# A slot's first four transposes moved ahead of the preceding slot's second product, and eight gate rows loaded sooner

## The chip, the cores and the metric

One core of one Trainium2 chip runs the whole kernel. The metric is the device time of one launch in microseconds (us). The kernel before the change has a median of 386.7 us over 3 runs (385.82 to 386.99).

The core's engines run side by side, each working through its own list of instructions in order and waiting on semaphores: TensorE (PE, matrix products and transposes into the eight banks of PSUM), VectorE (DVE), ScalarE (ACT), GpSimd (POOL) and SyncE (SP, which here only issues DMA transfers).

## The reference, cut to what matters

Three stages in a row on a batch of 2 x 768 tokens with 384 features:

```python
# 1: linear attention with a decaying 48x48 state per head (8 heads); x is [2, 768, 384] after it
state = w * state + k_t v_t;  y_t = r_t (state + u k_t v_t)
# 2: layer norm, then a hidden layer of 1536, added to x
x = x + relu(((x - mu) / sqrt(var + 1e-6) * g_ln) @ w_ch1) @ w_ch2
# 3: a mixture of 8 experts with a hidden layer of 1024
logits = x @ w_gate;  local = sigmoid(x @ w_local)
e[s] = argmax(logits[s]) if s == 0 or local[s] < 0.5 else e[s-1]
out[s] = softmax(logits[s])[e[s]] * (relu(x[s] @ w1[e[s]]) @ w2[e[s]])
```

## The kernel before, in words

Tokens are worked in 12 tiles of 128. Weights and activations are split into a high part (rounded to fp32r) and a low part (the difference, in the code `hi` and `lo`), and each product is three: high by high, low by high, high by low.

**First stage and hidden layer.** Two tiles are a group; there are six groups (0 to 5). On TensorE a group (`group`) makes eight blocks of the first product (`hidden`, L1033, pairs q = 0 to 7), with the attention products of later tiles between them, and then the second product for each of its two tiles (`rows_out`, L933 to L935). Each block q of the first product goes to one of two PSUM banks in turn. ScalarE makes its high part (L731), VectorE its low part (L1560), and only then may TensorE write block q + 2 into that bank. So block 2 of a group waits for VectorE's low part of block 0. GpSimd works meanwhile on the attention inputs of later tiles (`decays`, `rows`, `ends`).

**Gates.** The nine gate products of a token tile (eight experts and the local gate) are made on VectorE in `gates` (L1668): one `scalar_tensor_tensor` of 128 x 384 with an accumulated sum for each gate row, from the finished tile `x2` and the gate rows `wgr` broadcast to all partitions. VectorE's list is written out by hand, and gates are put in where it is thought to have time. For tile 0 the first five are at the start of group 1, ahead of `hidden(1, 0)`; for every later even tile the first four are in `rows_done`, between `turned` and `residual(g, 1)`.

**The gate rows** are loaded by SyncE in one transfer of nine rows (L469) into the first part of `stage`. That buffer held the pieces of `w_ch1` and `w_ch2` before; so the load waits for the semaphores `lo_v` and `lo_p`, by which VectorE and GpSimd tell that the low parts of all pieces are made. On SyncE's queue it stands behind the loads of tiles 4 and 5 and ahead of the stores of `x2`.

**Experts.** Tokens are gathered into slots of 128 that belong to one expert. Two early slots run beside the routing; then up to 18 slots (numbered from 0) run in a list that is cut off when no slot is live any more: with these inputs slots 0 to 13 are. From slot 9 on each slot's parts for the next one stand in an `If` on a value read from a table. In slot s TensorE does, in this order:

- `turn_rows(s+2)`: three transposes of gathered rows into bank 0 (L1318)
- `hidden_e(s+1, 0)`: nine products for the first half of the next slot's inner rows, into bank 2 (L1331, L1335, L1338)
- `turn_hidden(s)`: eight transposes of this slot's inner rows `he`, four into bank 4 and four into bank 5 (L1348)
- `hidden_e(s+1, 1)`: nine products for the other half of the next slot's inner rows, into bank 3
- `rows_out_e(s)`: the slot's second product, 24 matmuls into bank 6 (L1359, L1363, L1367)

Before four transposes are written into bank 4 or 5, `turn_hidden` waits for `he_ready` (ScalarE has made that half of `he`, L880) and for `heT_ready`, which counts VectorE's low parts (L1945): these read the same bank.

ScalarE in slot s (`slot`, L892 and after): the rows of slot s + 2 out of bank 0 (`turned_rows`, L872), the high parts of the two halves of the transposed rows (L902), two pieces of the next expert's weights rounded if its expert is new (`prepare`, L811), both halves of `he` for slot s + 1 (`hidden_rows`, L880), and two more pieces (L811).

VectorE in slot s: the low part of the rows of slot s + 2 (`turned_rows`, L1915), the low parts of the two halves of the transposed rows (L1945), two low parts of pieces if they are due (`prepare`, L1923), the output rows scaled (L1954, which waits for the end of `rows_out_e(s)`), and two more low parts of pieces if they are due (L1923). In slot 0 the code of the routing (`main_parts`) and `rest_e(1, EP)` (L1630) stand ahead of this list.

Of the kernel before, what the change touches and what calls it, by code (L numbers as in the profile page):

```python
# [15 lines left out]
P = 128  # L16
B, H, S, D = 2, 8, 768, 48
DM = H * D
# [9 lines left out]
F1 = 4 * DM  # L28
# [3 lines left out]
NG = NT // G  # L32
E = 8
# [19 lines left out]
LO_V = 2, 3, 5  # L53
LO_P = 5
GATED = (NG - 2) * G + 1
NSPENT = 6
# [56 lines left out]
def build_program(nc, consts, w_heads, u_row, r_t, k_t, r_rows, k_rows, v_rows, g_cols, w_ch1, w_ch2,  # L113
# [4 lines left out]
    with ExitStack() as ctx:  # L118
# [3 lines left out]
        def sem(name):  # L122
            return ctx.enter_context(nc.semaphore(name))
# [11 lines left out]
        ident = const("ident")  # L135
# [13 lines left out]
        at = WB + NT * DM  # L149
# [113 lines left out]
        p_got_e, p_slot_e = late([3, NEARLY]), late([NEARLY])  # L263
        xe = [xg[i].rearrange("p (k t) -> p k t", k=KD) for i in range(NEARLY)]
        heT_e = late([KF2, P])
        wgr = stage[:, 0:(E + 1) * DM]
        spent = [stage[:, (E + 1 + i) * DM:(E + 2 + i) * DM] for i in range(NSPENT)]

        parts_e = parts[:].rearrange("p (b w c) -> p b w c", b=2, w=2)

# [9 lines left out]
        s_zero, s_scan, s_wk, s_wr, s_we, s_uw, s_ng, s_eps = sems("s_zero s_scan s_wk s_wr s_we s_uw s_ng s_eps")  # L280
        rkT_ready, coef_mm = sems("rkT_ready coef_mm")
        s_pair, s_k1, s_hi0, s_wc = sem("s_pair"), sem("s_k1"), sem("s_hi0"), sem("s_wc")
        s_mean0, s_k2, s_gr, s_spent = sem("s_mean0"), sem("s_k2"), sem("s_gr"), sem("s_spent")
        s_v = [sem(f"s_v{u}") for u in range(2)]
        s_piece = [sem(f"s_piece{i}") for i in range(NPIECE)]
        s_warm = sem("s_warm")
# [95 lines left out]
        def when(eng, live, step):  # L382
            if live is None:
                step()
            elif live is not False:
                with eng.If(live > 0):
                    step()
# [11 lines left out]
        def _(sp):  # L399
# [17 lines left out]
            def load(c, u):  # L417
                load_turned(c, u)
                load_rows(c, u)
# [42 lines left out]
                sp.wait_ge(x2_ready, t + 1)  # L462
                sp.dma_start(x2_dram[bass.ds(t * P, P), :], x2[u]).then_inc(x2_out[u], 16)

            for u in range(2):
                load(4 + u, u)
            sp.wait_ge(lo_v, len(LO_V))
            sp.wait_ge(lo_p, LO_P)
            sp.dma_start(wgr, gate_rows.to_broadcast([P, (E + 1) * DM])).then_inc(s_gr, 16)  # L469
            for u in range(2):  # L470
                store(u, u)
            with sp.Fori(1, NG - 2) as g:
# [204 lines left out]
        def _(act):  # L677
# [194 lines left out]
                act.activation(xnT_hi[:, :, s % 2 * P:(s % 2 + 1) * P],  # L872
                               bk[0][:, 0:DM].rearrange("p (k t) -> p k t", k=KD), ACT.Copy).then_inc(xgT_hi_ready, 1)

            def hidden_rows(s):
                for half in range(2):
                    act.wait_ge(he_mm, 2 * s + half + 1)
                    if half == 0:
                        act.wait_ge(*((heT_mm, 2 * s) if s else (heeT_mm, 2 * NEARLY)))
                    act.activation(he[:, half * 512:(half + 1) * 512], bk[2 + half][:], ACT.Relu).then_inc(he_ready, 1)  # L880
# [12 lines left out]
            def slot(s, live):  # L893
                if s + 2 < NSLOT:
                    when(act, live, lambda: turned_rows(s + 2))
                if s + 1 < NSLOT:
                    read_name(s + 1)
                for half in range(2):
                    act.wait_ge(heT_mm, 2 * s + half + 1)
                    if half == 0:  # L900
                        act.wait_ge(*((ye_mm, s) if s else (yee_mm, NEARLY)))
                    act.activation(heT_hi[:, 4 * half:4 * half + 4, :].rearrange("p a t -> p (a t)"), bk[4 + half][:],  # L902
                                   ACT.Copy).then_inc(heT_hi_ready, 1)
                if s + 1 < NSLOT:
                    prepare(name[s + 1], range(EP))
                when(act, live, lambda: hidden_rows(s + 1))
                if s == 0:
                    round_e(1, EP + 1)
                else:
                    prepare(name[s], range(EP, 2 * EP))  # L910
# [10 lines left out]
        def _(pe):  # L921
# [399 lines left out]
            def hidden_e(s, e, half):  # L1321
                b = e if isinstance(e, int) else e & 1
                if half == 0:
                    pe.wait_ge(xgT_hi_ready, s + 1)
                pe.wait_ge(e_hi[0], e * EP + (half + 1))
                if s >= 1:
                    pe.wait_ge(he_ready, 2 * s + half - 1)
                u = slice(s % 2 * P, (s % 2 + 1) * P)
                hi, lo = (lambda k, w=w: e_cols(b, w, half * F1 + k * 512, 512) for w in range(2))
                for k in range(KD):  # L1330
                    pe.matmul(bk[2 + half][:], xnT_hi[:, k, u], hi(k), start=k == 0, stop=False)  # L1331
                if half == 0:
                    pe.wait_ge(xgT_ready, s + 1)
                for k in range(KD):
                    pe.matmul(bk[2 + half][:], xnT_lo[:, k, u], hi(k), start=False, stop=False)  # L1335
                pe.wait_ge(e_lo[0], e * EP + (half + 1))
                for k in range(KD):
                    mm = pe.matmul(bk[2 + half][:], xnT_hi[:, k, u], lo(k), start=False, stop=k == KD - 1)  # L1338
                mm.then_inc(he_mm, 1)

            def turn_hidden(s):
                for half in range(2):
                    pe.wait_ge(he_ready, 2 * s + half + 1)
                    if s >= 1:
                        pe.wait_ge(heT_ready, 2 * s + half - 1)
                    for f in range(4):
                        at = (4 * half + f) * P
                        mm = pe.transpose(bk[4 + half][:, f * P:(f + 1) * P], he[:, at:at + P], ident)  # L1348
                    mm.then_inc(heT_mm, 1)

            def rows_out_e(s, e):
                b = e if isinstance(e, int) else e & 1
# [26 lines left out]
            def slot(s, live):  # L1379
                if s + 1 < NSLOT:  # L1380
                    expert[s + 1] = pe.value_load(slot_tab[0:1, 0, s + 1:s + 2], min_val=0, max_val=E - 1)

                def ahead():
                    if s + 2 < NSLOT:
                        turn_rows(s + 2)
                    hidden_e(s + 1, expert[s + 1], 0)

                when(pe, live, ahead)
                turn_hidden(s)
                when(pe, live, lambda: hidden_e(s + 1, expert[s + 1], 1))  # L1390
                if s == 0:
                    lanes_main()
                rows_out_e(s, expert[s])
# [4 lines left out]
            hidden_e(0, 0, 0)  # L1398
            turn_rows(1)
            hidden_e(0, 0, 1)  # L1400
            pe.wait_ge(rt_v, RT_TABLES)
            live_slots(pe, slot)


        @block.vector
        def _(dve):
# [253 lines left out]
            def gates(t, columns):  # L1660
                dve.wait_ge(x2_ready, t + 1)
                if t == 0:
                    dve.wait_ge(s_gr, 16)
                for e in columns:
                    n = t * (E + 1) + e
                    if n >= NSPENT:
                        dve.wait_ge(s_spent, n - NSPENT + 1)
                    dve.scalar_tensor_tensor(spent[n % NSPENT], x2[t % 2], 1.0, wgr[:, e * DM:(e + 1) * DM],  # L1668
                                             ALU.mult, ALU.mult, accum_out=lg[:, t, e:e + 1]).then_inc(s_spent, 1)

            def group(g, ends=True):
                t0, t1 = (g - 1) * 2, (g - 1) * 2 + 1
                gates(t0, range(0 if g == 1 else 4, 5))
                hidden(g, range(0, 1))
                if not ends:
                    coefs(g * 2 + 2, 0)
                masked(g * 2 + 2, bk[0:2], scT[0])
                gates(t0, range(5, 7))
                hidden(g, range(1, 2))
                if ends:  # L1680
                    coefs(g * 2 + 2, 0)
                gates(t0, range(7, 8))
                hidden(g, range(2, 3))
                if ends:
                    new_state(g * 2 + 2, 0, bk[3])
                rows_of(g * 2 + 2, 0, bk[4])
                if not ends:
                    coefs(g * 2 + 3, 1)
                masked(g * 2 + 3, bk[0:2], scT[0])
                if ends:  # L1690
                    coefs(g * 2 + 3, 1)
                gates(t0, range(8, E + 1))
                hidden(g, range(3, 4))
                gates(t1, range(0, 1))
                hidden(g, range(4, 5))
                if ends:
                    new_state(g * 2 + 3, 1, bk[3])
                rows_of(g * 2 + 3, 1, bk[4])
                means(g + 1)
                gates(t1, range(1, 2))  # L1700
                hidden(g, range(5, NHP))
                gates(t1, range(2, E + 1))
                rows_done(g)

            def rows_done(g):
                if isinstance(g, int) and g == NG - 2:
                    dve.wait_ge(s_rest, 16)
                    flags(0)
                residual(g, 0)
                turned(g + 1)  # L1710
                if 0 < g < NG - 2:
                    gates(g * 2, range(0, 4))
                elif g == NG - 2:
                    gates(g * 2, range(0, 6))
                residual(g, 1)
                scales(g + 1)
                if g == NG - 2:
                    gates(g * 2, range(6, E + 1))
# [333 lines left out]
```

## Time and profile before

| what | value |
|---|---|
| median of 3 runs | 386.7 us |
| the profiled execution's own time | 387.67 us |
| its span in the profile | 385.8 us |
| TensorE busy | 372.7 us, 97% of the span |
| VectorE busy | 281.7 us, 73% |
| ScalarE busy | 155.4 us, 40% |
| GpSimd busy | 136.2 us, 35% |
| share of the chain that ended last | TensorE 89%, VectorE 6% |
| granted TensorE clock | full in nearly every slice |

The span is what the profile shows from the first to the last instruction. Every engine has a busy time; what matters is which engine the others wait for, and in which stretch. Here TensorE is busy nearly all the time, so the places where it sits idle are few.

### The profile page before, as it was taken

How to read it: one execution, taken by the hardware profiler on the slowest of the kernel's cores; microseconds unless marked ns; L12 is line 12 of the kernel's file. 1: busy time of each engine (PE TensorE's matmuls, PEld its weight loads, DVE VectorE, ACT ScalarE, POOL GpSimd, SP SyncE). 2: the span in 40 equal slices, each digit the busy share in tenths (PEclk: the TensorE clock that was granted, in tenths of full speed). 3: DMA queues.
4: the chain of work that ended last, by engine and by line, in shares of the span. 5: the costliest groups of instructions: out<-in, count | busy, mean ns of one | idle time of the engine just before them, and what ended most of it. 6: DMA issues, size and time to landing. Idle time of an engine off the chain costs nothing.

```text
span 385.8 us, 8869 instructions
## 1 busy us (share of the span) xinstructions
PE 372.7 (97%) x3056; PEld 338.9 (88%) x3056; DVE 281.7 (73%) x630; ACT 155.4 (40%) x281; POOL 136.2 (35%) x114
## 2 busy tenths in 40 slices
PE   8999989999999999999999999999999999999992
PEld 6889989999999999999999656789999999999981
DVE  7899769897898788769868568698646853647440
ACT  6556312212231321241441254368525852555520
POOL 2999772931760470100004006303332233223231
PEclk9999999999999999999999999999999999999997
DMA  7995633300511331400028495798875297101111
GB/s 216 337 338 167 198 129 111 113 20 25 169 44 42 109 109 41 165 3 22 20 83 292 136 309 141 262 369 308 297 274 160 76 286 286 39 22 48 20 47 42
DMA packets 32778, 56.67 MB, mean 147 GB/s; under 512 B 3277, under 2 KB 20339, under 8 KB 32608
## 3 DMA queue, kind: packets, MB, share of 16 engines
q1 hardware_dynamic: 30432, 49.84, 39.5%
q0 software_dynamic: 2304, 6.30, 5.6%
q8 instruction: 23, 0.38, 0.4%
q14 instruction: 19, 0.16, 0.1%
HBM read 51.41 MB, written 5.51 MB: 148 GB/s over the span
## 4 chain that ended last, share of the span: by engine, by line
PE 89%; DVE 6%; issue 2%; DMA 1%; ACT 1%; POOL 0%; SPq 0%; DVEq 0%; POOLq 0%; ACTq 0%
PE bank L1033 17%; PE bank L933 7%; PE bank L935 7%; PE bank L934 6%; PE bank L1359 5%; PE bank L1331 5%; PE bank L1367 5%; PE bank L1363 5%; PE bank L1338 5%; PE bank L1335 5%; PE bank L1348 3%; PE bank L1260 3%; PE bank L1237 3%; PE bank L948 3%; PE bank L979 2%
## 5 line engine op out<-in xcount | busy, mean ns | idle before, releaser
L1033 PE MATMUL bank<-xnT_hi,parts 128*128 128x256 f32 x432 | 65.5, 288 | 1.7 <-DVE parts L1560 1.4
L1033 PEld LDWEIGHTS bank<-xnT_hi,parts 128*128 128x128 f32 x432 | 56.6, 191 | 4.0 <-DVE parts L1560 1.9
L731 ACT ACTIVATE parts<-bank 128x512 fp32r<-128x512 f32 x36 | 21.5, 597 | 91.9 <-PE bank L1033 91.8
L1668 DVE SCALAR_TENSOR_TENSOR stage<-stage 128x384 f32<-128x384 f32 x81 | 56.4, 738 | 0.2
L665 POOL DMA_INDIRECT out_y<-late x14 | 20.5, 1461 | 93.9 <-DVE late L1954 93.9
L933 PE MATMUL bank<-parts 128*128 128x384 f32 x144 | 49.2, 342 | 0.0
L935 PE MATMUL bank<-parts 128*128 128x384 f32 x144 | 48.3, 335 | 0.0
L934 PE MATMUL bank<-parts 128*128 128x384 f32 x144 | 48.2, 334 | 0.0
L811 ACT ACTIVATE parts<-stage (+1 forms) x32 | 46.2, 1485 | 0.2 <-DMA stage<-in_w 0.2
L1923 DVE TENSOR_TENSOR parts<-stage,parts x24 | 41.1, 1755 | 4.9 <-ACT parts L811 4.2
L1033 PE MATMUL bank<-xnT_lo,parts 128*128 128x256 f32 x216 | 37.3, 282 | 0.0
L1560 DVE SCALAR_TENSOR_TENSOR parts<-bank,parts 128x512 fp32r<-128x512 f32 x36 | 24.8, 690 | 17.0 <-ACT parts L731 16.6
L572 POOL TENSOR_TENSOR arena<-arena,coef 128x384 f32<-128x384 f32 x12 | 13.0, 1080 | 62.3 <-DVE coef L1450 62.0
L1954 DVE TENSOR_SCALAR late<-bank,late 128x384 f32<-128x384 f32 x14 | 8.6, 618 | 32.6 <-PE bank L1367 32.5
L658 POOL DMA_INDIRECT late<-x_rows,late x18 | 22.3, 1240 | 28.2 <-DVE late L1880 23.0
L1033 PEld LDWEIGHTS bank<-xnT_lo,parts 128*128 128x128 f32 x216 | 30.9, 191 | 0.0
L933 PEld LDWEIGHTS bank<-parts 128*128 128x128 f32 x144 | 27.1, 188 | 0.1
L934 PEld LDWEIGHTS bank<-parts 128*128 128x128 f32 x144 | 27.1, 188 | 0.0
L935 PEld LDWEIGHTS bank<-parts 128*128 128x128 f32 x144 | 27.0, 188 | 0.0
L1331 PE MATMUL bank<-parts,xnT_hi 128*128 (+1 forms) x84 | 26.6, 425 | 0.0
L902 ACT ACTIVATE heT_hi<-bank 128x512 fp32r<-128x512 f32 x28 | 15.2, 595 | 28.0 <-PE bank L1348 28.0
L1945 DVE TENSOR_TENSOR heT_lo<-bank,heT_hi 128x512 fp32r<-128x512 f32 x28 | 18.0, 684 | 11.3 <-ACT heT_hi L902 11.3
(257 smaller groups left out, 731.5 us busy)
## 6 DMA issues: line engine op xcount, KB each, us to landing
stage<-in_w SPq DMA_DIRECT2D x36, 768.0 KB, 7.2
stage<-in_w_ch SPq DMA_DIRECT2D x6, 768.0 KB, 8.6
arena<-in_k_t SPq DMA_DIRECT2D x12, 224.0 KB, 3.4
arena<-in_r_t SPq DMA_DIRECT2D x12, 224.0 KB, 3.0
arena<-in_v_rows SPq DMA_DIRECT2D x12, 192.0 KB, 4.3
arena<-in_k_rows SPq DMA_DIRECT2D x12, 192.0 KB, 3.3
x_rows<-stage SPq DMA_DIRECT2D x12, 192.0 KB, 1.9
arena<-in_r_rows SPq DMA_DIRECT2D x10, 192.0 KB, 3.3
```

The lines of the kernel that those rows point to most:

```text
L658: pool.indirect_dma_start(xg[s % XR], None, x2_dram, bass.IndirectOffsetOnAxis(take[:, s:s + 1], 0)).then_inc(s_xg[s % XR], 16)
L665: pool.indirect_dma_start(out, bass.IndirectOffsetOnAxis(give[:, s:s + 1], 0), yo[s % 2], None, bounds_check=T - 1, oob_is_err=False).then ...
L731: act.activation(hT_hi[:, 2 * q:2 * q + 2, :].rearrange("p a t -> p (a t)"), bk[6 + q % 2][:], ACT.Relu).then_inc(h_hi_ready, 1)
L811: act.activation(e_at(b, 0, j), e_stage(h, j), ACT.Copy).then_inc(e_hi[j // EP], 1)
L933: pe.matmul(out_, a_lo, b_hi, start=start, stop=False)
L934: pe.matmul(out_, a_hi, b_lo, start=False, stop=False)
L935: return pe.matmul(out_, a_hi, b_hi, start=False, stop=stop)
L1033: mm = pe.matmul(acc, w[:, k, at], x[:, k, :], start=start and k == 0, stop=stop and k == KD - 1, skip_group_check=first and q == 0)
L1331: pe.matmul(bk[2 + half][:], xnT_hi[:, k, u], hi(k), start=k == 0, stop=False)
L1560: dve.scalar_tensor_tensor(hT_lo[:, at, :].rearrange("p a t -> p (a t)"), bk[6 + q % 2][:], 0.0, hT_hi[:, at, :].rearrange("p a t -> p (a ...
L1668: dve.scalar_tensor_tensor(spent[n % NSPENT], x2[t % 2], 1.0, wgr[:, e * DM:(e + 1) * DM], ALU.mult, ALU.mult, accum_out=lg[:, t, e:e + 1] ...
L1923: dve.tensor_tensor(e_at(e & 1, 1, j), e_stage((e + 1) & 1, j), e_at(e & 1, 0, j).bitcast(F32), ALU.subtract).then_inc(e_lo[j // EP], 1)
```

## The change

In the slot list TensorE makes the four transposes of the first half of slot s + 1 (into bank 4) in slot s, between `hidden_e(s+1, 1)` and `rows_out_e(s)`. In slot s + 1 only the four transposes of the second half are left at the old place. For slot 0 they stand behind `hidden_e(0, 0, 1)`, ahead of the wait for the routing tables. ScalarE makes the first half of `he` for slot s + 1 ahead of the two pieces, the second half behind them.

The gate rows come in two transfers: eight rows into the third and fourth quarter of the buffer's first half as soon as VectorE has made the low part of piece 3 (and before the load of tile 5 is issued), the ninth at the old place. Four of tile 0's gates move from the start of group 1 to `rows_done` of group 0.

```diff
-        wgr = stage[:, 0:(E + 1) * DM]
-        spent = [stage[:, (E + 1 + i) * DM:(E + 2 + i) * DM] for i in range(NSPENT)]
+        wgr = [stage[:, 2 * F1 + e * DM:2 * F1 + (e + 1) * DM] for e in range(E)] + [stage[:, 0:DM]]
+        spent = [stage[:, (1 + i) * DM:(2 + i) * DM] for i in range(NSPENT)]
...
-            for u in range(2):
-                load(4 + u, u)
+            load(4, 0)
+            sp.wait_ge(lo_v, LO_V.index(3) + 1)
+            sp.dma_start(stage[:, 2 * F1:4 * F1], gate_rows[:, 0:E * DM].to_broadcast([P, E * DM])).then_inc(s_gr, 16)
+            load(5, 1)
             sp.wait_ge(lo_v, len(LO_V))
             sp.wait_ge(lo_p, LO_P)
-            sp.dma_start(wgr, gate_rows.to_broadcast([P, (E + 1) * DM])).then_inc(s_gr, 16)
+            sp.dma_start(wgr[E], gate_rows[:, E * DM:].to_broadcast([P, DM])).then_inc(s_g9, 16)
...
# ScalarE, slot(s, live)
+                when(act, live, lambda: hidden_rows(s + 1, range(1)))
                 if s + 1 < NSLOT:
                     prepare(name[s + 1], range(EP))
-                when(act, live, lambda: hidden_rows(s + 1))
+                when(act, live, lambda: hidden_rows(s + 1, range(1, 2)))
...
# TensorE
+            def turn_hidden(s, half):
+                pe.wait_ge(he_ready, 2 * s + half + 1)
+                if s >= 1:
+                    pe.wait_ge(heT_ready, 2 * s + half - 1)
+                for f in range(4):
+                    at = (4 * half + f) * P
+                    mm = pe.transpose(bk[4 + half][:, f * P:(f + 1) * P], he[:, at:at + P], ident)
+                mm.then_inc(heT_mm, 1)
...
+                def rest():
+                    hidden_e(s + 1, expert[s + 1], 1)
+                    turn_hidden(s + 1, 0)
+
                 when(pe, live, ahead)
-                turn_hidden(s)
-                when(pe, live, lambda: hidden_e(s + 1, expert[s + 1], 1))
+                turn_hidden(s, 1)
+                when(pe, live, rest)
...
             hidden_e(0, 0, 1)
+            turn_hidden(0, 0)
             pe.wait_ge(rt_v, RT_TABLES)
...
# VectorE
                 if t == 0:
                     dve.wait_ge(s_gr, 16)
+                    dve.wait_ge(s_g9, 16)
...
-                gates(t0, range(0 if g == 1 else 4, 5))
+                gates(t0, range(4, 5))
...
-                if 0 < g < NG - 2:
+                if g < NG - 2:
                     gates(g * 2, range(0, 4))
```

## Rows read from the trace of the kernel before

**Rows 1.** Waits of TensorE: who waited for whom, total, times, longest (us)

```profile
PE bank L1033 <- DVE parts L1560: 1.4, 1, 1.4
...
PE bank L1359 <- ACT heT_hi L902: 0.7, 1, 0.7
```

**Rows 2.** Timeline of VectorE, 31 to 58: start us, us, instruction, [idle before <- releaser]

```profile
31.90 2.08 DVE L1504 TENSOR_TENSOR parts<-stage,parts 128x1536 fp32r<-128x1536 f32 x1
...
51.30 0.62 DVE L1573 SCALAR_TENSOR_TENSOR stage<-bank,rstd,stage 128x384 f32<-128x384 f32 x1 [4.03 <-PE bank L935]
...
54.29 1.33 DVE L1668 SCALAR_TENSOR_TENSOR stage<-stage 128x384 f32<-128x384 f32 x1
...
57.47 0.68 DVE L1560 SCALAR_TENSOR_TENSOR parts<-bank,parts 128x512 fp32r<-128x512 f32 x1
```

**Rows 3.** Timeline of TensorE at 58

```profile
58.20 0.98 PE L1033 MATMUL bank<-xnT_hi,parts 128*128 128x256 f32 x6 [1.36 <-DVE parts L1560]
```

**Rows 4.** Engines between 47.26 and 51.30 (busy us, count; clock, DMA share, GB/s)

```profile
47.26:51.30 4.04, 4.04 (x26) 4.04 (x25) 0.01 (x2) 0.00 (x0) 3.96 (x5) 1.00 0.80 309
```

**Rows 5.** Timeline of VectorE: one gate beside a busy GpSimd, one beside an idle one

```profile
78.19 1.35 DVE L1668 SCALAR_TENSOR_TENSOR stage<-stage 128x384 f32<-128x384 f32 x1
...
83.80 0.54 DVE L1668 SCALAR_TENSOR_TENSOR stage<-stage 128x384 f32<-128x384 f32 x1
```

**Rows 6.** Timeline of SyncE: the issue of the gate rows

```profile
43.25 0.37 SPq L469 DMA_DIRECT2D stage<-in_gate_rows  x1
```

**Rows 7.** DMA issues: count, KB each, median us from issue to landing

```profile
arena<-in_v_rows SPq DMA_DIRECT2D x12, 192.0 KB, 4.3
...
stage<-in_gate_rows SPq DMA_DIRECT2D x1, 1728.0 KB, 9.4
```

**Rows 8.** Timeline of TensorE, slot 3

```profile
276.68 0.49 PE L1318 MATMUL bank<-cst,late 128*128 128x128 f32 x3
...
279.09 1.04 PE L1348 MATMUL bank<-cst,late 128*128 128x128 f32 x8
279.88 0.95 PE L1331 MATMUL bank<-parts,xnT_hi 128*128 x3
...
282.05 1.58 PE L1359 MATMUL bank<-parts,heT_hi 128*128 x8
```

**Rows 9.** Timeline of VectorE, end of slot 2 and slot 3

```profile
276.88 0.62 DVE L1954 TENSOR_SCALAR late<-bank,late 128x384 f32<-128x384 f32 x1 [3.70 <-PE bank L1367]
277.62 3.43 DVE L1923 TENSOR_TENSOR parts<-stage,parts  x2
...
281.43 1.28 DVE L1945 TENSOR_TENSOR heT_lo<-bank,heT_hi 128x512 fp32r<-128x512 f32 x2
```

**Rows 10.** The line L1945: duration min/median/max in ns

```profile
L1945 DVE TENSOR_TENSOR heT_lo<-bank,heT_hi x28: 680/682/692, 253.0 to 374.7; 128x512 fp32r<-128x512 f32 x28
```

**Rows 11.** Timeline of ScalarE, slot 3

```profile
280.70 0.61 ACT L880 ACTIVATE late<-bank 128x512 f32<-128x512 f32 x1
```

**Rows 12.** Timeline of VectorE, slot 0

```profile
252.95 1.28 DVE L1945 TENSOR_TENSOR heT_lo<-bank,heT_hi 128x512 fp32r<-128x512 f32 x2
```

**Rows 13.** Timeline of TensorE, slot 0

```profile
253.04 0.50 PE L1373 MATMUL bank<-late 128*128 128x54 bf16 x12
```

**Rows 14.** Timeline of VectorE, slot 12

```profile
367.30 1.28 DVE L1945 TENSOR_TENSOR heT_lo<-bank,heT_hi 128x512 fp32r<-128x512 f32 x2
```

**Rows 15.** Timeline of TensorE, slots 12 and 13

```profile
367.91 1.58 PE L1359 MATMUL bank<-parts,heT_hi 128*128 x8
...
372.10 1.04 PE L1348 MATMUL bank<-cst,late 128*128 128x128 f32 x8
373.81 1.65 PE L1359 MATMUL bank<-parts,heT_hi 128*128 x8 [0.67 <-ACT heT_hi L902]
```

**Rows 16.** Chain of waits at the start of slot 13's second product

```profile
372.74 0.61 ACT heT_hi L902
373.34 0.46 issue
```

More of the change, by code:

```diff
@@ L282, in build_program @@
         s_pair, s_k1, s_hi0, s_wc = sem("s_pair"), sem("s_k1"), sem("s_hi0"), sem("s_wc")
-        s_mean0, s_k2, s_gr, s_spent = sem("s_mean0"), sem("s_k2"), sem("s_gr"), sem("s_spent")
+        s_mean0, s_k2, s_gr, s_g9, s_spent = sem("s_mean0"), sem("s_k2"), sem("s_gr"), sem("s_g9"), sem("s_spent")
         s_v = [sem(f"s_v{u}") for u in range(2)]
@@ L873, in turned_rows, with hidden_rows @@
                                bk[0][:, 0:DM].rearrange("p (k t) -> p k t", k=KD), ACT.Copy).then_inc(xgT_hi_ready, 1)
-            def hidden_rows(s):
-                for half in range(2):
+            def hidden_rows(s, halves=range(2)):
+                for half in halves:
                     act.wait_ge(he_mm, 2 * s + half + 1)
@@ L1339, in hidden_e @@
                 mm.then_inc(he_mm, 1)
[L1341 to L1349, printed above, removed]
+            def turn_hidden(s, half):
[6 more added lines that the diff above has]
+                mm.then_inc(heT_mm, 1)
             def rows_out_e(s, e):
@@ L1667, in gates @@
                         dve.wait_ge(s_spent, n - NSPENT + 1)
-                    dve.scalar_tensor_tensor(spent[n % NSPENT], x2[t % 2], 1.0, wgr[:, e * DM:(e + 1) * DM],
+                    dve.scalar_tensor_tensor(spent[n % NSPENT], x2[t % 2], 1.0, wgr[e],
                                              ALU.mult, ALU.mult, accum_out=lg[:, t, e:e + 1]).then_inc(s_spent, 1)
```

## The prediction

> **What bounds the kernel now.** I read the waits of TensorE first, because the page gives it 97% of the span: the reader is to see that in the parts that the change touches it waits twice only, once for VectorE's low part L1560 and once for ScalarE's L902 [rows 1]. Next the timelines of VectorE, TensorE, GpSimd and SyncE around the first wait [rows 2 to 7], to see what stands ahead of the low part. Then the timelines of the slots, engine beside engine [rows 8 to 16]: TensorE goes from block to block without a gap there, so moving its work gains nothing by itself, and the question is only which new wait the new order makes.
>
> **Part 1: the gates of tile 0.** Block 2 of group 1 could start at 58.20 - 1.36 = 56.84 and starts at 58.20, 0.05 after VectorE's low part of block 0, which runs from 57.47 to 58.15 [rows 2, 3]. Ahead of it VectorE makes five gates, from 54.29 on, and a low part can't be earlier than these: 3.2 us. Ahead of them it sat idle for 4.03 us, from the end of `turned` at 47.27 to the residual at 51.30 [rows 2]. The change puts four gates into that gap and leaves one.
>
> Would they fit? The eight rows can be issued once the low part of piece 3 is made, at 31.90 + 2.08 = 33.98 [rows 2], 9.3 us before the old issue at 43.25 [rows 6]; with the whole load's 9.4 us [rows 7] they land by about 43.4. SyncE has to wait there for VectorE, but the load of tile 5 behind it has its own later waits. The ninth row is issued where the nine were, at about 43.25, and every gate of tile 0 now waits for it. It is 192 KB; a load of that size lands in 4.3 us [rows 7], so at 47.6, 0.3 after VectorE is free.
>
> The price of a gate depends on GpSimd. It is 0.54 us with GpSimd idle and 1.35 beside it [rows 5], and GpSimd is busy 3.96 of the 4.04 us of the gap [rows 4]. So four gates take from 4 x 0.48 = 1.9 us (starts 0.48 apart where it is idle) to 4 x 1.28 = 5.1 us (from start to start, 1.35 less its overlap). I take the upper one, the row nearest to the place: 47.6 + 5.1 = 52.7 against a residual that could go at 51.30. The residual and the five small operations behind it (`scales`) took 54.29 - 51.30 = 3.0 us, and a contended gate is 1.2 to the next start [rows 2]; so the low part of block 0 starts near 52.7 + 3.0 + 1.2 = 56.9 if all goes as badly as before. But GpSimd's list is finite and is not longer than before, so some of those stalls are used up in the gap; I take 56.6. With 0.68 for it and 0.05 TensorE then restarts at 57.3 and not at 58.20. Gain: **0.9 us**. Bounds: 1.36, the whole wait, if it fits; and 2 us lost, if the ninth row should land as late as the nine did (52.65) and everything behind it with it.
>
> The Trainium skill ("GPSIMD Engine Reference", section "1. Specifications") says that GpSimd's SBUF interfaces are shared with VectorE and contend with its instructions of two SBUF inputs, which a gate is. By this rule the gap with GpSimd at work is a poor place; without it the gates would fit and the gain would be 1.36. The trace agrees with the rule (1.35 against 0.54), and the sum above goes by the rows.
>
> **Part 2: the slots.** TensorE's work in a slot stays the same: 3 transposes, 9 products, 4 transposes, 9 products, 4 transposes, 24 products. What changes is a condition. The four transposes into bank 4 now stand ahead of slot s's second product, and need bank 4 free: VectorE's low part of slot s, first half. Before, that low part was needed only by the second eight matmuls of the second product (L1363), 1.4 us into it, or by the transposes of the next slot.
>
> Slot 3 shows both sides. TensorE: the four transposes that stay take half of 279.88 - 279.09 = 0.79, so 0.40, and everything behind them is 0.40 earlier; the moved ones could start at 282.05 - 0.40 = 281.65 [rows 8]. VectorE: the end of slot 2 is seen at 276.88; the scaling, two low parts of pieces and the rows of slot 5 come before the low part wanted, which starts at 281.43 [rows 9] and takes 0.69 [rows 10]; with 0.05 to TensorE [rows 2, 3] that is 282.17. TensorE waits for 0.52 us. VectorE's list isn't changed, and all of it hangs on the end of the slot before, as TensorE's work does. So the wait returns whenever the pieces are due, and each adds to the end, as nothing else is slack on TensorE.
>
> VectorE makes two pieces just before this low part in slots 2, 3, 6, 7, 10 and 12; the same sum gives 0.52 to 0.57 for each, the last being 367.30 + 0.69 + 0.05 - (367.91 - 0.40) = 0.53 [rows 14, 15]. In slot 0 it is the routing that makes it late: 252.95 + 0.74 = 253.69 against the start at 253.04, at which the second block is over, so 0.65 [rows 12, 13]. Together (six from 0.52 to 0.57, and 0.65) 3.9 us. A first group of matmuls after a wait also runs slower, 1.65 against 1.58 for eight [rows 15], so 7 x 0.07 = 0.5. **Cost 4.4 us.** In the other slots (1, 4, 5, 8, 9, 11) VectorE has no two pieces there, and ScalarE's high part can now be made at the start of the slot, since its transposes are already there; no wait. Bounds: from 0.40 each (the low part 0.12 faster) to 0.75 each, so 2.8 to 5.3 in all.
>
> ScalarE's part costs nothing: the first half of `he` for slot 4 was made from 280.70 to 281.31 [rows 11], behind both high parts of slot 3; it now stands behind one of them, 0.5 earlier, so it ends at 280.8, 0.8 before the transposes could want it at 281.65. Where pieces are due it now comes ahead of them. Their two pieces begin at the same time as before, since one operation of 0.6 (the high part of the first half) is gone from the place and one came. The cover that hides it is `hidden_e(s+1, 1)`, 2.1 us. The second half of `he` is needed only a slot later.
>
> **Part 3: the end.** Slot 13 has no next slot. Before, TensorE made eight transposes (372.10) and started the second product at 373.81, 0.67 after the transposes were over [rows 15]. Now four remain, and the high part of the first half needs only the end of slot 12. Of the 1.71 us the chain gives 0.61 to ScalarE and 0.46 to issue [rows 16], the latter a TensorE that jumps over the code left out. I take four transposes gone, **0.4 us gained**; bounds 0 (the jump covers all) and 0.9 (the jump is hidden too). The Trainium skill ("Runtime: NRT & Kernel Launch", section "Instruction fetch mechanics") says that a taken branch to code outside the window waits for a fetch. By it the 0.46 stays, and the end gains 0.4; otherwise it would be 0.9. No more than that hangs on it: the slots with an `If` were as long as those without.
>
> **The sum.** - 0.9 + 4.4 - 0.4 = +3.1 us. The profiled execution's 387.67 us becomes 390.8. It lay 1.0 above the median of the runs shown, so against that: 386.7 + 3.1 = **389.8 us**, 0.8% slower.
>
> **The rivals.**
> - *The waits are shorter, the gains whole.* VectorE's chain or TensorE's path is off by 0.15 us for each slot. Cost 2.8, gains 1.36 and 0.9: +0.5, 387.2 us, not to be told from no change. Against it: seven separate slots show the same margin within 0.13 us. Chance 0.08.
> - *No wait at all in the slots (the other side).* One mechanism: bank 4's low part is done before TensorE comes. It decides at 0.52 us: if VectorE's way from the end of a slot to that low part (276.88 to 282.12) is that much shorter, the cost of part 2 is zero. Then -1.36 - 0.4 = -1.8: 384.9 us. For it: half of the slots have this slack. Against it: the five operations in between stand in VectorE's list in any case, and nothing of them is removed. Chance 0.07.
> - *The ninth row is late.* All gates of tile 0 wait for it, and the residual behind them, so VectorE's whole list. If it lands at 52.65 as before, the low part of block 0 is 2 us later than in the old order: 0.9 of gain becomes 2 of loss, and the time is 392.7. For it: it is behind three loads of tile 5. Against it: eight ninths of the bytes have gone before. Chance 0.08.
> - *The forecast:* 0.77.
>
> A measurement of this kernel can tell about 0.3%, 1.2 us, from no change. The forecast's own range, with the bounds of its terms (+0.6 to +5 at the ends, hardly all at once), is 388.3 to 391.3. With the rivals up to 2 in 10 left out the range is 387.4 to 391.4. Slower by over 0.3%: forecast and late row, 0.85; within 0.3%: 0.08; faster: 0.07.
>
> **What would show it.** In the profile after: a group L1348 with idle time before it, released by VectorE's L1945, seven times, about 0.5 us each (slots 0, 2, 3, 6, 7, 10, 12); slots of 10.1 us in place of 9.5 there, and of 9.5 elsewhere. At group 1 four L1668 between 47 and 53 of over a microsecond each, and TensorE's wait for L1560 at about 0.4 in place of 1.36. At the end, 1.3 us from the first transpose of slot 13 to its second product. It would be wrong if TensorE's L1348 shows no idle time in slots 2 and 3, or if VectorE sits idle ahead of the first gate for more than a microsecond.

## The result and the profile after

The changed kernel takes 391.0 us (median of 4 runs, 390.77 to 391.97) against 386.85 (4 runs, 385.82 to 387.81): ratio 1.0106, 95% interval 1.0087 to 1.0125, so 4.1 us slower. The forecast was 389.8, which is 3.1 slower. The profiled execution has a span of 390.2 us, 4.4 more than before.

These two lines of the page give the busy times and the chain that ended last. TensorE's share of the chain falls from 89 to 75%, VectorE's rises from 6 to 13%:

```profile
PE 374.5 (96%) x3056; PEld 338.1 (87%) x3056; DVE 285.1 (73%) x630; ACT 156.8 (40%) x281; POOL 137.6 (35%) x114
...
PE 75%; DVE 13%; issue 5%; DVEq 2%; DMA 1%; ACT 1%; SPq 1%; POOL 0%; POOLq 0%; ACTq 0%
```

The waits of TensorE (who waited for whom: us in total, times, longest). The first line is new: seven waits of the transposes for VectorE's low part. The last one answers to the first of [rows 1]:

```profile
PE bank L1350 <- DVE heT_lo L1953: 3.6, 7, 0.6
...
PE bank L1361 <- ACT heT_hi L904: 0.8, 1, 0.8
PE bank L1036 <- DVE parts L1567: 0.6, 1, 0.6
```

Slot 2 in TensorE's timeline (start, us, instruction, idle before and releaser). From the last products of the second block (271.76) to the transposes behind them it is 1.34 us:

```profile
267.52 0.49 PE L1321 MATMUL bank<-cst,late 128*128 128x128 f32 x3
...
269.93 0.60 PE L1350 MATMUL bank<-cst,late 128*128 128x128 f32 x4
...
271.76 0.84 PE L1341 MATMUL bank<-parts,xnT_hi 128*128 x3
273.10 0.63 PE L1350 MATMUL bank<-cst,late 128*128 128x128 f32 x4 [0.50 <-DVE heT_lo L1953]
273.48 1.66 PE L1361 MATMUL bank<-parts,heT_hi 128*128 x8
...
277.77 0.49 PE L1321 MATMUL bank<-cst,late 128*128 128x128 f32 x3
```

VectorE meanwhile did the output rows, two pieces, the rows of slot 4, and only then the low parts, the first of which (0.68) ends at 272.95. It is the list of [rows 9], with the same distances:

```profile
267.72 0.62 DVE L1962 TENSOR_SCALAR late<-bank,late 128x384 f32<-128x384 f32 x1 [0.32 <-PE bank L1369]
268.46 3.43 DVE L1931 TENSOR_TENSOR parts<-stage,parts  x2
271.80 0.55 DVE L1923 TENSOR_TENSOR xnT_lo<-bank,xnT_hi 128x384 fp32r<-128x384 f32 x1
272.27 1.28 DVE L1953 TENSOR_TENSOR heT_lo<-bank,heT_hi 128x512 fp32r<-128x512 f32 x2
```

In slot 5 no pieces are due at that place. TensorE goes through with 0.69 from the last products to the transposes, and the slot is 9.56 us long (297.57 to 307.13), against 10.25 for slot 2 and against 9.53 for slot 5 before:

```profile
297.57 0.49 PE L1321 MATMUL bank<-cst,late 128*128 128x128 f32 x3
...
301.81 0.85 PE L1341 MATMUL bank<-parts,xnT_hi 128*128 x3
302.50 0.60 PE L1350 MATMUL bank<-cst,late 128*128 128x128 f32 x4
302.85 1.65 PE L1361 MATMUL bank<-parts,heT_hi 128*128 x8
...
307.13 0.49 PE L1321 MATMUL bank<-cst,late 128*128 128x128 f32 x3
```

There VectorE made that low part early, from the transposes made in the slot before:

```profile
297.76 0.62 DVE L1962 TENSOR_SCALAR late<-bank,late 128x384 f32<-128x384 f32 x1 [0.32 <-PE bank L1369]
298.61 0.56 DVE L1923 TENSOR_TENSOR xnT_lo<-bank,xnT_hi 128x384 fp32r<-128x384 f32 x1 [0.23 <-ACT xnT_hi L874]
299.34 0.69 DVE L1953 TENSOR_TENSOR heT_lo<-bank,heT_hi 128x512 fp32r<-128x512 f32 x1 [0.17 <-ACT heT_hi L904]
```

The gates of tile 0 in VectorE's timeline, and then the wait behind them in TensorE's:

```profile
47.23 0.59 DVE L1676 SCALAR_TENSOR_TENSOR stage<-stage 128x384 f32<-128x384 f32 x1 [0.22 <-DMA stage<-in_gate_rows]
...
47.75 1.36 DVE L1676 SCALAR_TENSOR_TENSOR stage<-stage 128x384 f32<-128x384 f32 x1
...
49.04 1.36 DVE L1676 SCALAR_TENSOR_TENSOR stage<-stage 128x384 f32<-128x384 f32 x1
...
50.33 1.62 DVE L1676 SCALAR_TENSOR_TENSOR stage<-stage 128x384 f32<-128x384 f32 x1
...
51.89 0.61 DVE L1580 SCALAR_TENSOR_TENSOR stage<-bank,rstd,stage 128x384 f32<-128x384 f32 x1
...
55.22 1.34 DVE L1676 SCALAR_TENSOR_TENSOR stage<-stage 128x384 f32<-128x384 f32 x1
...
56.49 0.68 DVE L1567 SCALAR_TENSOR_TENSOR parts<-bank,parts 128x512 fp32r<-128x512 f32 x1
```

```profile
57.23 0.98 PE L1036 MATMUL bank<-xnT_hi,parts 128*128 128x256 f32 x6 [0.64 <-DVE parts L1567]
```

Before slot 0 four transposes now stand ahead of the rows of slot 2, and at the end four are left. TensorE's timeline:

```profile
246.78 0.60 PE L1350 MATMUL bank<-cst,late 128*128 128x128 f32 x4
247.21 0.49 PE L1321 MATMUL bank<-cst,late 128*128 128x128 f32 x3
...
376.94 0.60 PE L1350 MATMUL bank<-cst,late 128*128 128x128 f32 x4
378.37 1.65 PE L1361 MATMUL bank<-parts,heT_hi 128*128 x8 [0.83 <-ACT heT_hi L904]
```

**Where the 4.6 us lie.** The same instruction's start in both traces, after less before; what each stretch adds:

| TensorE's instruction | before | after | difference | the stretch adds |
|---|---|---|---|---|
| group 1, block 0 | 51.10 | 50.84 | -0.26 | -0.26 |
| group 1, block 2 [rows 3] | 58.20 | 57.23 | -0.97 | -0.71 |
| first product for slot 0 | 242.87 | 241.98 | -0.89 | +0.08 |
| rows of slot 2 turned (slot 0 begins) | 247.67 | 247.21 | -0.46 | +0.43 |
| slot 13's transposes [rows 15] | 372.10 | 376.94 | +4.84 | +5.30 |
| slot 13's second product [rows 15] | 373.81 | 378.37 | +4.56 | -0.28 |

Behind the last row the execution after is 0.2 us shorter, which gives the 4.4 of the spans.

### The profile page after: what moved, and what is told of

It is laid out like the page before. It is cut to its first block, busy times and chain, and to the rows that moved or that the text cites. A ratio compares the mean times of both kernels' runs of the same rounds, so it can differ in the third digit from the quotient of the medians.

```text
span 390.2 us, 8879 instructions
## 1 busy us (share of the span) xinstructions
PE 374.5 (96%) x3056; PEld 338.1 (87%) x3056; DVE 285.1 (73%) x630; ACT 156.8 (40%) x281; POOL 137.6 (35%) x114
## 4 chain that ended last, share of the span: by engine, by line
PE 75%; DVE 13%; issue 5%; DVEq 2%; DMA 1%; ACT 1%; SPq 1%; POOL 0%; POOLq 0%; ACTq 0%
PE bank L1036 17%; PE bank L936 5%; PE bank L938 5%; PE bank L937 5%; PE bank L1361 5%; PE bank L1369 5%; PE bank L1365 5%; PE bank L1263 3%; PE bank L1240 3%; PE bank L951 3%; PE bank L1350 2%; PE bank L1334 2%; PE bank L1341 2%; PE bank L1338 2%; PE bank L982 2%
## 5 line engine op out<-in xcount | busy, mean ns | idle before, releaser
L1676 DVE SCALAR_TENSOR_TENSOR stage<-stage 128x384 f32<-128x384 f32 x81 | 59.2, 771 | 0.4 <-DMA stage<-in_gate_rows 0.2
L1036 PEld LDWEIGHTS bank<-xnT_hi,parts 128*128 128x128 f32 x432 | 56.6, 191 | 3.2 <-DVE parts L1567 1.1
L904 ACT ACTIVATE heT_hi<-bank 128x512 fp32r<-128x512 f32 x28 | 16.7, 599 | 22.4 <-PE bank L1350 16.1
```

The lines of the kernel that those rows point to most:

```text
L1036: mm = pe.matmul(acc, w[:, k, at], x[:, k, :], start=start and k == 0, stop=stop and k == KD - 1, skip_group_check=first and q == 0)
```

## The experiments

Each ratio is to the kernel before, run on the same chip in the same rounds (387.31 us median in the first four, 387.04 in the last four, 29 runs each). The changed kernel itself was not run again, so a comparison with it goes by the ratios (its own is 1.0106). Edits are cut and shown against the changed kernel unless the text says otherwise.

**The transposes alone.** The gate rows and gates are as before the change.

```diff
-            load(4, 0)
-            sp.wait_ge(lo_v, LO_V.index(3) + 1)
-            sp.dma_start(stage[:, 2 * F1:4 * F1], gate_rows[:, 0:E * DM]...
...
-                gates(t0, range(4, 5))
+                gates(t0, range(0 if g == 1 else 4, 5))
```

> The moved transposes alone; gate rows and gates as before the change. Theory (TensorE waits in seven slots for bank 4, and the gates save 0.7 us): the seven waits of L1349 or thereabouts stay, group 1's wait is 1.36 us again, and the time is 0.7 above the changed kernel, about 391.7. Rival (the gates moved are worth nothing, because their price beside GpSimd eats it): equal to the changed kernel, 391.0.

Measured: 391.31 us (390.98 to 392.89), ratio 1.0107, 1.0087 to 1.0128. In the trace the seven waits are there, and group 1's is back at 1.51:

```profile
PE bank L1348 <- DVE heT_lo L1950: 3.5, 7, 0.6
PE bank L1034 <- DVE parts L1565: 1.5, 1, 1.5
```

So the transposes carry the whole loss. The times don't tell theory and rival on the gates apart: 0.3 us lie between the medians, none between the ratios. The rows do so for one execution each (a wait of 1.51 against 0.64).

**The gates alone.** The slots are as before the change.

```diff
-                def rest():
-                    hidden_e(s + 1, expert[s + 1], 1)
-                    turn_hidden(s + 1, 0)
+                turn_hidden(s)
+                when(pe, live, lambda: hidden_e(s + 1, expert[s + 1], 1))
```

> The gate rows and the four gates moved alone; the slots as before the change. Theory: group 1's wait falls from 1.36 to about 0.64 us, nothing else moves, 0.7 below the kernel before: 386.1. Rival (no gain): 386.85.

Measured: 386.5 us (384.99 to 387.28), ratio 0.998, 0.9964 to 0.9996: 0.8 us faster, where the theory had 0.7. The interval lies only just below 1, and a later run of nearly the same kernel (the ninth row not waited for, below) doesn't repeat the gain. The 13 slots from the first to the last take 124.41 us (246.84 to 371.25), before 124.43.

```profile
PE bank L1361 <- ACT heT_hi L904: 0.7, 1, 0.7
PE bank L1035 <- DVE parts L1562: 0.6, 1, 0.6
```

**Another bank.** In the changed kernel odd slots use bank 7 for their first four transposes, and the wait for VectorE's low part goes back to the slot that last used the same bank.

```diff
+        def turned_bank(s, half):
+            return bk[5] if half else bk[7 if s % 2 else 4]
...
-                if s >= 1:
-                    pe.wait_ge(heT_ready, 2 * s + half - 1)
+                if s == 1 and half == 0:
+                    pe.wait_ge(rt_v, RT_PARTS)
+                if half == 1 and s >= 1:
+                    pe.wait_ge(heT_ready, 2 * s)
+                if half == 0 and s >= 2:
+                    pe.wait_ge(heT_ready, 2 * s - 3)
...
-                    mm = pe.transpose(bk[4 + half][:, ...
+                    mm = pe.transpose(turned_bank(s, half)[:, ...
```

> The changed kernel, but the first four transposes of odd slots go to bank 7, those of even slots to bank 4, so that each has a slot more before its bank is wanted again. Theory (the wait is for the bank that VectorE still reads): all seven waits of the moved transposes go, 0.68 to 0.78 us each from start to start, 4.8 in all: 386.2. Rival (the new order costs by itself: three changes from transposes to products in a slot in place of two, more jumps): no wait in the rows, but the time stays within 1 us of 391.0.

Measured: 386.89 us (385.3 to 388.33), ratio 0.9994, 0.9977 to 1.0011. All seven waits are gone, as the theory has it, though VectorE's low part is as late as ever. The rows are TensorE's and then VectorE's in slot 2. The transposes start at 271.87, 0.18 after the start of the low part that they had to wait for in the changed kernel:

```profile
266.94 0.49 PE L1324 MATMUL bank<-cst,late 128*128 128x128 f32 x3
...
271.87 0.60 PE L1357 MATMUL bank<-cst,late 128*128 128x128 f32 x4
...
276.50 0.49 PE L1324 MATMUL bank<-cst,late 128*128 128x128 f32 x3
```

```profile
271.69 1.28 DVE L1960 TENSOR_TENSOR heT_lo<-bank,heT_hi 128x512 fp32r<-128x512 f32 x2
```

Every slot is 9.56 long except slot 0, and the 13 take 124.70 us (247.40 to 372.10). So of the 5.30 us of the table 129.73 - 124.70 = 5.03 are the waits and 0.27 is the new order itself, 0.00 to 0.03 a slot: the rival's cost is there, but small.

**VectorE's order.** The changed kernel keeps its banks; the low part of the next slot's first half is made between the two pieces at a slot's end.

```diff
+                    prepare(name[s], range(EP, EP + 1))
+                when(dve, live, lambda: turned_low(s + 1, 0))
+                if s:
+                    prepare(name[s], range(EP + 1, 2 * EP))
...
             main_parts()
+            turned_low(0, 0)
             rest_e(1, EP)
```

> The changed kernel with banks as they are, but VectorE makes the low part of the next slot's first half between the two pieces at a slot's end, and in slot 0 ahead of the last piece of expert 1. Theory (what makes the low part late is its place in VectorE's list, behind two pieces and one set of rows): the low part is ready 3.1 us after the end of the slot before, the transposes come at 4.9, all seven waits go: 386.2. Rival (the bank's reuse costs whatever the order, or ScalarE's high part becomes the late one): waits stay or turn up with ScalarE as releaser, over 389.

Measured: 386.15 us (385.25 to 388.58), ratio 0.9973, 0.9955 to 0.999. The low part comes between the pieces, and TensorE goes through; the 13 slots take 124.66 us (249.22 to 373.88). VectorE, slot 2:

```profile
269.66 1.76 DVE L1931 TENSOR_TENSOR parts<-stage,parts  x1
271.33 0.68 DVE L1948 TENSOR_TENSOR heT_lo<-bank,heT_hi 128x512 fp32r<-128x512 f32 x1
271.94 1.75 DVE L1931 TENSOR_TENSOR parts<-stage,parts  x1
```

Two cures, one of the bank and one of the order, each take 5.0 to 5.1 us out of the slots. The cause is shown: a bank still read by VectorE, whose read stands late in its list.

In this profiled execution, the slowest of its twelve, the gates came late: the ninth row landed 6.4 us after its issue, VectorE sat idle for it, and TensorE's wait in group 1 was 1.6 us. The lines are the DMA issue (KB, us to landing) and VectorE's first gate:

```profile
stage<-in_gate_rows SPq DMA_DIRECT2D x1, 192.0 KB, 6.4
```

```profile
50.80 1.55 DVE L1676 SCALAR_TENSOR_TENSOR stage<-stage 128x384 f32<-128x384 f32 x1 [2.75 <-DMA stage<-in_gate_rows]
```

**The ninth row not waited for.** This is the kernel with the gates alone, and the edit is against it; the first eight wait for their load and for GpSimd's low parts.

```diff
                     dve.wait_ge(s_gr, 16)
-                    dve.wait_ge(s_g9, 16)
+                    dve.wait_ge(lo_p, LO_P)
                 for e in columns:
+                    if t == 0 and e == E:
+                        dve.wait_ge(s_g9, 16)
```

> The gates alone moved (slots as before), and only the ninth gate waits for the ninth row; the first eight wait for their own load and for GpSimd's low parts, whose buffer they write into. In one execution of the kernel with VectorE's new order the ninth row took 6.4 us and VectorE sat idle 2.75 us for it. Theory (a late ninth row now and then takes the gain back): VectorE never waits over 0.3 us ahead of the first gate, and the median is 0.2 to 0.5 below the 386.5 of the gates alone. Rival (the row is in time nearly always): equal within 0.1.

Measured: 386.71 us (386.24 to 387.75), ratio 0.9993, 0.9979 to 1.0007. The ninth row took 5.7 us here and VectorE no longer waited for it: its gates start at 46.97. But TensorE's wait was 0.8. The theory failed, as no gain can be measured, neither against the kernel before nor against the gates alone (0.998). The first gate, started 0.23 sooner than with the gates alone, took 1.09 us beside GpSimd and not 0.72, and the low part came at 56.73 and not at 56.59.

**Three gates in the gap.** This is the last kernel with two gates left for group 1.

```diff
-                gates(t0, range(4, 5))
+                gates(t0, range(3 if g == 1 else 4, 5))
...
-                    gates(g * 2, range(0, 4))
+                    gates(g * 2, range(0, 4 if g else 3))
```

> As the one before, with three gates in the gap in place of four and two at the start of group 1. Theory (in the gap a gate costs 1.29 us beside GpSimd and the fourth delays the residual by 0.85): the residual is in time, the two gates left start near 54.2 and cost 1.3 and 0.5, block 0's low part starts at 56.0, and TensorE's wait falls from 0.62 to under 0.2 us: 0.4 below four gates. Rival (GpSimd's work only moves: what isn't contended in the gap is contended behind it): wait and time equal to four gates.

Measured: 386.98 us (385.4 to 388.91), ratio 1.0009, 0.9992 to 1.0026. The rival was right: TensorE's wait is 0.79, as in the run before. The residual is in time at 51.06, but the first of the small operations is now slow (1.04 us for 2 columns), and the low part starts at 56.65, against 56.73 in the run before:

```profile
51.06 0.62 DVE L1575 SCALAR_TENSOR_TENSOR stage<-bank,rstd,stage 128x384 f32<-128x384 f32 x1 [0.64 <-PE bank L937]
...
51.78 1.04 DVE L1529 TENSOR_TENSOR sq<-rstd 128x2 f32<-128x2 f32 x1
...
56.65 0.68 DVE L1562 SCALAR_TENSOR_TENSOR parts<-bank,parts 128x512 fp32r<-128x512 f32 x1
```

**A later low part.** The changed kernel with one more operation, its result unused, ahead of the low parts in each slot.

```diff
+                dve.tensor_tensor(x2T[:].rearrange("p k t -> p (k t)"), cst[:, 0:DM], cst[:, 0:DM], ALU.mult)
                 for half in range(2):
                     dve.wait_ge(heT_hi_ready, 2 * s + half + 1)
```

> The changed kernel with one more VectorE operation (128 x 384, two inputs from SBUF, its result unused) in every slot, just ahead of the low parts of the transposed rows. Theory (the low part is the releaser in seven slots and has slack of over 2 us in the other six): each of the seven waits grows by one operation's step of 0.47 us and no other slot grows: 3.3 us slower than the changed kernel, 394.3. Rival (TensorE's loss comes from something in all slots): all 14 slots grow, 6 us or more; or none does, 391.0.

Measured: 395.12 us (394.45 to 396.19), ratio 1.0208, 1.0189 to 1.0228: 1.0 percentage point or 4 us above the changed kernel. In the trace the same seven waits grow, five of them from 0.50 to 0.96 or so, and the other slots stay at 9.56; all 13 take 133.34 us (247.92 to 381.26), 3.6 more. The excess over 3.3 lies in slot 12, whose wait is 1.35: there VectorE's pieces also started 0.51 late, behind a wait for nothing that the profile shows. Another 0.5 us of this execution lies ahead of the slots. There the ninth row landed late again, VectorE sat idle for it, and TensorE's wait in group 1 was 1.1 and not 0.6.

```profile
PE bank L1350 <- DVE heT_lo L1954: 7.3, 7, 1.4
```

```profile
274.75 0.63 PE L1350 MATMUL bank<-cst,late 128*128 128x128 f32 x4 [0.97 <-DVE heT_lo L1954]
```

```profile
48.48 0.79 DVE L1676 SCALAR_TENSOR_TENSOR stage<-stage 128x384 f32<-128x384 f32 x1 [1.31 <-DMA stage<-in_gate_rows]
```

**The early transposes against none, once nothing waits.** VectorE has its new order, and only the ninth gate waits for the ninth row.

```diff
+                when(dve, live, lambda: turned_low(s + 1, 0))
...
+                    if t == 0 and e == E:
+                        dve.wait_ge(s_g9, 16)
```

> The moved transposes with VectorE's new order and the gates moved with only the ninth waiting for the ninth row. Theory by the traces (13 slots 0.02 longer each without any wait, four transposes made ahead of slot 0, 0.43, and 0.3 to 0.4 saved at the end): 0.3 slower than the kernel with the gates alone and the same waits. Rival (the early transposes give something once nothing waits for bank 4): faster than that kernel by 0.2 or more.

Measured: 386.88 us (385.29 to 387.47), ratio 0.9986, 0.997 to 1.0002, against 386.71 and 0.9993 for the gates alone with the same waits. The medians and the ratios differ in sign, and the sign is left open. In the two traces the rows add to 0.3 us longer, as the theory has it (+0.43 ahead of slot 0, +0.25 in the 13 slots, -0.37 at the end). Either way the early transposes bring nothing that can be told from zero. Of all kernels the gates alone (0.998) and VectorE's order with four gates (0.9973) are the two whose interval lies below 1, both by less than 0.3%.

## Why the prediction was right, and where its sizes were not

**The new wait in seven slots: right.** It is on TensorE's L1350, released by VectorE's low part, in slots 0, 2, 3, 6, 7, 10 and 12 and in no other, and the three kernels that take its cause away lose it. The way from the end of a slot to the low part was 4.55 us before and after (267.72 to 272.27), as assumed.

**Its size: 4.4 foreseen, 5.30 measured.** For slot 2 0.63 was foreseen (0.56 and 0.07) and 0.69 came. The release is the mis-sized term: I took 0.05 us from VectorE's end to TensorE's next start, from a product that had waited [rows 2, 3]; the transposes started at 273.10, 0.15 after 272.95. The slower restart was 0.03 or 0.04 and not 0.07. The 0.07 had been read off a product behind a wait (1.65 against 1.58 for eight), but it is no mark of a wait: slot 5 waits for nothing and shows 1.65 too, in a product right behind transposes. Slots 10 and 12, with an `If`, lost 0.78 and 0.75, since the second product began 0.46 and 0.44 after the transposes and not 0.38. That makes 5.03. The other 0.27 is the order itself, which I had at nothing: in slot 5 two groups of four transposes take 0.70 between them against 0.79 for eight, but the second product, now behind transposes and no more behind products, takes 1.49 for its first eight and not 1.42, and the products between the transposes take 2.17 and not 2.14.

**The end: one step was wrong.** "I take four transposes gone, 0.4 us gained" counts TensorE's work as less at the end and forgets that the four made ahead of slot 0 are added there, 0.43 (246.78 to 247.21), a term that the prediction put at nothing. The 0.4 itself was well sized: from slot 13's transposes to its second product it was 1.71 before and 1.32 or 1.33 in all five experiments with the new order. In the profiled execution of the changed kernel it was 1.43, which is why the table has only 0.28 there. So the end gives no net gain: +0.15 in the table, +0.05 by the five, where the prediction had -0.4.

The gain is also not shown to be that of the four transposes. ScalarE's high part began with the end of slot 12, 0.38 sooner behind the first transpose than before, and in nine of the ten traces TensorE's second product starts 0.46 after the end of that part's first half, whether eight transposes stand ahead of it or four. That the 0.46 is a jump over code, as the prediction has it, no run tests; the profile says only "issue". In the changed kernel's own execution it was 0.57, and the chain there names the second half of the high part (377.69 to 378.29), for which the first four products don't wait by the code; why it was so is open. The chain there (start, us, what):

```profile
377.69 0.60 ACT heT_hi L904
378.29 0.08 issue
```

In the kernel with the other bank, the same stretch is as before [rows 16]:

```profile
372.36 0.60 ACT heT_hi L907
372.96 0.46 issue
373.43 1.70 PE bank L1368 x8
```

So the upper bound of 0.9, by which the 0.46 would vanish, was not met in any trace.

**The gates: right in mechanism.** Foreseen: the ninth row 0.3 us late, here 0.22; gates at 1.28 each beside GpSimd, here 1.29 from the second on; gain 0.9, here 0.71 in the rows. The run with the gates alone gives 0.8 by its times (0.2 to 1.4 by its interval), but the later run with the same gates and less waiting gave a ratio of 0.9993, whose interval reaches 1. So the gain is shown in the rows and only just in the times. TensorE's wait was to be 0.4 and was 0.64. The restart at 57.23 is near the 57.3 foreseen only because this execution was 0.26 early ahead of group 1. The residual came 0.85 late (51.89 against 51.30 - 0.26), not 1.4, because the first gate took only 0.52 to the next start; the last took 1.56.

Two of these figures are luck. The ninth row was issued 0.6 later than assumed (43.83) and landed in 3.3 and not 4.3. And the 56.6 for the low part rested on the thought that GpSimd's stalls would be used up in the gap. They were not: the residual and the small operations took 3.33 us behind the gap (3.0 before) and the last gate 1.27 (taken as 1.2). The residual, half a microsecond earlier than summed, made up for that.

The rival of a late ninth row was true in two of the five profiled executions whose gates all wait for it, at 0.9 us (VectorE's new order) and 0.5 us (the later low part) and not at 2.9.

**The sum.** In the profiled executions the rows add to 4.56 where 3.1 was forecast: 0.9 more from the slots, 0.55 from the end (0.10 of it this execution's 1.43 in place of 1.33), 0.27 from the gates with the stretch behind them (-0.71 + 0.08 against -0.9), less 0.26 by which the two executions differ ahead of group 1, which no run here explains. The medians differ by 4.1, which is 1.0 above the forecast.

## What to carry to other kernels

When work is moved ahead on an engine that never idles, it can't gain more than the places where that engine waits, and each move has to be paid for by a new condition: list what must have been read out of the buffer before the moved writer may start, and compare both paths from their last common event. Here that comparison of two rows gave the loss in seven places before the run. If the order is wanted all the same, a second buffer or an earlier reader takes the whole wait away. And work that is moved is never gone: what one end gains, the other pays.

## What the runs showed of the hardware

VectorE's gates, which read two inputs from SBUF, and GpSimd's products slow each other down. In the gap a gate from the second on takes 1.29 to 1.56 us to the next start and not 0.48, and GpSimd's products of 112 x 512 take 1.60 and not 1.28, those of 128 x 384 1.33 and not 1.01. The residual, which reads a PSUM bank, keeps its 0.61 to 0.62 in every trace. So the contention was only pushed about: in the six executions with three or four gates in the gap and a first gate from 46.94 to 47.28, the low part started between 56.49 and 56.73.

```profile
49.95 1.60 POOL L530 TENSOR_TENSOR arena<-arena 112x512 f32<-112x512 f32 x1
```

A load of 192 KB behind the same three loads took 3.3, 4.0, 3.9, 6.4, 5.7, 3.9, 5.0 and 4.1 us in eight executions. VectorE stood still for it 0.22, 0, 0.25, 2.75 and 1.31 us in the five whose gates all wait for it: a wait placed just before the usual landing costs in some executions.
